# Squared-ReLU layer behind pooled attention and a soft mixture: joins spread over the steps, row additions moved to GpSimd, and another order of the first sixteen units

## The reference

```python
def _attn_ref(q, k, v):          # 8 batches, 8 heads, 576 tokens, head size 64
    k_p, v_p = ...               # keys and values averaged in groups of 8
    scores = scale * np.matmul(q, k_p.transpose(0, 1, 3, 2))
    ...
    return np.matmul(attn, v_p)

def _moe_ref(x, phi, w1, w2):    # soft mixture: x is (4608, 512), 32 slots in all
    logits = x @ phi
    ...
    return c @ slot_out          # c: (4608, 32), slot_out: (32, 512)

def _moe2_ref(x, w_in, w_out, s, b):   # w_in (512, 2048), w_out (2048, 512)
    h = x @ w_in
    r = np.maximum(h, 0.0)
    g = s * (r * r) + b
    return g @ w_out
```

## Time and profile before

| what | us |
|---|---|
| median of 3 runs | 681.96 (676.74 to 683.46) |
| profiled execution, its own time | 676.74 |
| its span | 674.9 |
| PE busy in the span | 637.7 (94%) |
| DVE, ACT, POOL busy | 480.2, 450.0, 126.1 |

### The profile page before, as it was taken

How to read it: one execution, slowest core, us unless ns; L and a number is a source line. 1 busy time by engine, 2 the same in 40 slices (tenths; PEclk the granted TensorE clock), 3 DMA queues, 4 the chain that set the end, 5 groups by cost and what they waited for, 6 DMA issues and landing times.

```text
span 674.9 us, 16536 instructions
## 1 busy us (share of the span) xinstructions
PE 637.7 (94%) x6466; PEld 550.2 (82%) x6466; DVE 480.2 (71%) x791; ACT 450.0 (67%) x753; POOL 126.1 (19%) x127
## 2 busy tenths in 40 slices
PE   7788999999998889989999999999999999999996
PEld 7566777776753247869999999999999999999996
DVE  5757575665344738875878777877787778777886
ACT  1576777776411279975777777777777777777771
POOL 3899786622110010002200000000000000000000
PEclk9799999999998999998999999999999999999999
DMA  9788969573589930000100000000000000000001
GB/s 336 229 265 295 362 211 404 164 306 128 190 311 432 424 140 1 1 0 16 64 18 32 18 18 29 22 24 16 31 16 31 16 31 16 31 16 31 17 33 48
DMA packets 25236, 80.49 MB, mean 119 GB/s; under 512 B 6496, under 2 KB 14688, under 8 KB 22368
## 3 DMA queue, kind: packets, MB, share of 16 engines
q1 hardware_dynamic: 25184, 79.76, 31.7%
HBM read 70.32 MB, written 9.44 MB: 118 GB/s over the span
## 4 chain that ended last, share of the span: by engine, by line
PE 40%; DVE 9%; issue 5%; ACT 3%; DVEq 0%; ACTq 0%
PE bank L1814 13%; PE bank L1816 12%; PE bank L1815 12%; DVE lo_sb L1303 3%; PE bank L1734 3%; ACT hi_sb L995 2%; DVE a_sb L1286 2%; DVE o_sb L1316 2%; DVE a_sb L1290 1%; PE bank L1776 1%; DVE a_sb L1292 0%; DVE o_sb L1355 0%; ACT r_sb L972 0%; ACT t_late L957 0%; DVE o_sb L1308 0%
## 5 line engine op out<-in xcount | busy, mean ns | idle before, releaser
L1303 DVE TENSOR_TENSOR lo_sb<-a_sb,hi_sb 128x896 fp32r<-128x896 f32 x128 | 140.2, 1096 | 66.2 <-ACT hi_sb L995 66.2
L995 ACT ACTIVATE hi_sb<-a_sb 128x896 fp32r<-128x896 f32 x128 | 121.9, 953 | 91.9 <-PE bank L1816 88.9
L1814 PE MATMUL bank<-w_hi,hi_sb 128*128 128x256 f32 x384 | 113.1, 294 | 7.0 <-DVE lo_sb L1303 6.9
L1815 PE MATMUL bank<-w_lo,hi_sb 128*128 128x256 f32 x384 | 108.8, 283 | 0.0
L1816 PE MATMUL bank<-w_hi,lo_sb 128*128 128x256 f32 x384 | 108.7, 283 | 0.0
L979 ACT ACTIVATE a_sb<-r_sb 128x512 f32<-128x512 f32 x144 | 91.1, 633 | 6.5
L972 ACT ACTIVATE r_sb<-bank 128x512 f32<-128x512 f32 x144 | 83.7, 581 | 2.9 <-PE bank L1734 2.9
L1814 PEld LDWEIGHTS bank<-w_hi,hi_sb 128*128 128x128 f32 x384 | 73.9, 192 | 11.7 <-DVE lo_sb L1303 10.9
L1815 PEld LDWEIGHTS bank<-w_lo,hi_sb 128*128 128x128 f32 x384 | 74.0, 193 | 0.0
L1816 PEld LDWEIGHTS bank<-w_hi,lo_sb 128*128 128x128 f32 x384 | 73.8, 192 | 0.0
L1816 PE MATMUL bank<-t_early,lo_sb 128*128 128x256 f32 x256 | 72.8, 284 | 0.0
(11 more groups left out here) (185 smaller groups left out, 1341.5 us busy)
## 6 DMA issues: line engine op xcount, KB each, us to landing
early_third<-in_moe_w_dram SPq DMA_DIRECT2D x6, 2048.0 KB, 13.8
kvbuf<-in_k_dram SPq DMA_DIRECT2D x12, 768.0 KB, 5.8
kvbuf<-in_v_dram SPq DMA_DIRECT2D x12, 768.0 KB, 6.7
out_dram<-o_sb SPq DMA_DIRECT2D x36, 256.0 KB, 2.3
qbuf<-in_q_dram SPq DMA_DIRECT2D x8, 1024.0 KB, 8.5
early<-in_moe_w_dram SPq DMA_DIRECT2D x4, 2048.0 KB, 12.2
late<-in_moe_w_dram SPq DMA_DIRECT2D x4, 2048.0 KB, 19.7
win_sb<-in_moe_w_in_dram SPq DMA_DIRECT2D x4, 1024.0 KB, 5.5
```

The costliest lines, as they stand in the source:

```text
L995: act.activation(hi_sb[:, n % 2, :], a_sb[:, n % ARING, P:2 * CH], ACT.Copy).then_inc(hi_ready, 1)
L1303: dve.tensor_tensor(lo_sb[:, n % 2, :], a_sb[:, n % ARING, P:2 * CH], hi_sb[:, n % 2, :].bitcast(F32), ALU.subtract).then_inc(lo_ready, 1)
L1814: pe.matmul(acc, hi, rhs_hi, start=opens, stop=False, skip_group_check=True)
L1815: pe.matmul(acc, hi, rhs_lo, start=False, stop=False, skip_group_check=True)
```

## The change

- **Joins and row additions.** The five joins of a half stand one behind each of steps 2 to 6 of the next half. The two additions of `row_b` leave DVE; POOL makes them, each when the join before it is done. In the last half DVE still makes the very last one.
- **Units.** In its round u ACT makes `relu` and `square` up to u + lead(u) before `high_easy(u)`, not behind it. PE issues h up to u + lead(u) + 2 behind unit u.
- **Combos.** POOL makes the first two sets, DVE the other six; the places of the sets' high and low parts move by a unit or two.
- **Row sum.** `sum_rows` goes from behind step 2 of half 0 to behind step 5, `scale_row` on ACT from step 4 to step 7, and what waits for the row on POOL with it.

```diff
-    POOL_COMBOS = 1
+    POOL_COMBOS = 2
...
             for m in range(MT):
-                sp.wait_ge(out_first, m + 1)
+                sp.wait_ge(out_ready, m + 1)
...
+            def add_row(m):
+                pool.tensor_tensor(o_sb[:, m, :], o_sb[:, m, :], row_b, ALU.add).then_inc(out_ready, 1)
+
+            def add_rows(c, odd, final):
+                pool.wait_ge(joined, c * JOINS + 3)
+                add_row(2 * odd)
+                if not final:
+                    pool.wait_ge(joined, c * JOINS + JOINS)
+                    add_row(2 * odd + 1)
...
-                pool.tensor_tensor(o_sb[:, m, :], o_sb[:, m, :], row_b, ALU.add).then_inc(out_first, 1)
+                add_row(m)
+            with pool.Fori(0, HALVES - 2, 2) as c:
+                add_rows(c, 0, False)
+                add_rows(c + 1, 1, False)
+            add_rows(HALVES - 2, 0, False)
+            add_rows(HALVES - 1, 1, True)
...
-                    if first and k == 4:
+                    if first and k == KP - 1:
                         scale_row()
...
-            high_at = {1: 0, 3: 1, 5: 2, 7: 3, 9: 4, 11: 5, 13: 6}
+            high_at = {1: 0, 2: 1, 4: 2, 6: 3, 8: 4, 11: 5, 14: 6}
             for u in range(F2C):
-                if u:
-                    high_easy(u)
                 while begun <= u + lead(u):
                     relu(begun, begun, bank[4 + begun % 2] if begun < F2C else bank[7], begun >= 2)
                     square(begun, begun, begun >= ARING)
                     begun += 1
+                if u:
+                    high_easy(u)
...
-                    if not first:
-                        for n in JOIN_AT[k]:
-                            join(c - 1, 1 - odd, n)
-                        if k in ADD_AT:
-                            add_row(c - 1, 1 - odd, ADD_AT.index(k))
+                    if not first and 2 <= k < 2 + JOINS:
+                        join(c - 1, 1 - odd, k - 2)
...
-            made_at = {1: 1, 3: 2, 5: 3, 7: 4, 9: 5, 11: 6, 13: 7}
-            low_at = {2: 0, 4: 1, 6: 2, 8: 3, 10: 4, 12: 5, 14: 6}
+            made_at = {2: 2, 4: 3, 6: 4, 8: 5, 10: 6, 13: 7}
+            low_at = {1: 0, 3: 1, 5: 2, 7: 3, 9: 4, 12: 5, 14: 6}
...
-            for n in range(3):
+            for n in range(JOINS):
                 join(HALVES - 1, 1, n)
-            join(HALVES - 1, 1, 3)
-            add_row(HALVES - 1, 1, 0)
-            join(HALVES - 1, 1, 4)
-            add_row(HALVES - 1, 1, 1)
+            dve.wait_ge(joined, HALVES * JOINS)
+            dve.tensor_tensor(o_sb[:, MT - 1, :], o_sb[:, MT - 1, :], row_b, ALU.add).then_inc(out_last, 1)
...
-                    while issued <= u + lead(u + 2) + 2:
+                    while issued <= u + lead(u) + 2:
                         hidden_at(issued)
                         issued += 1
...
-                    if first and k == 2:
+                    if first and k == 5:
                         sum_rows()
```

More of the change, by code:

```diff
@@ L356, in pooled_attention_soft_moe_squared_relu_kernel @@
         out_ready = sem("out_ready")
-        out_first = sem("out_first")
+        out_last = sem("out_last")
         o_dve = sem("o_dve")
@@ L734, in _ @@
                 for m in range(2):
-                    sp.wait_ge(out_ready, 2 * c + m + 1)
+                    if c == HALVES - 1 and m == 1:
+                        sp.wait_ge(out_last, 1)
+                    else:
+                        sp.wait_ge(out_ready, MT + 2 * c + m + 1)
                     sp.dma_start(tile_rows(MT + 2 * c + m), o_sb[:, 2 * (c % 2) + m, :]).then_inc(stored[2 * (c % 2) + m], 16)
@@ L1261, in combos @@
                 n = COMBOS * (k - POOL_COMBOS)
[L1262 to L1267, removed]
+                dve.wait_ge(t_hi_ready, k - 1)
+                dve.wait_ge(t_lo_ready, k - 1)
                 dve.tensor_tensor(t_raw_of(k, T1), raw_block(k, 0, 0), raw_block(k, 0, 1), ALU.subtract).then_inc(t_made, 1)
@@ L1345, in join @@
                 last.then_inc(joined, 1)
[L1347 to L1355, removed]
             def steps(c, odd, first, final):
```

## The result

The changed kernel takes 699.43 us (median of 4 runs, 696.41 to 702.8) where the kernel before took 679.93 us on the same chip (676.74 to 683.46): a ratio of 1.0287, with a 95% interval of 1.0211 to 1.0363. It is 19.5 us slower; the prediction said 20.9 us slower, 703 us.

What follows compares the result with a forecast made beforehand. PE, 94% busy, was taken as the bound, waiting only for DVE's low part; +6.3, +1.2, +11.5, -0.6 and +2.5 us on 676.74 gave 697.6 us, or 703 us against the median, range 690 to 712.

Steps and rivals of the forecast that it cites:

- Part 1: Joins and additions in the steady halves: PE waits for DVE, +0.42 us a half, +6.3 us over 15 halves.
- The first turn: Behind step 4, POOL's addition makes DVE stand 1.0 us after join 2; PE waits 0.7 us at step 5.
- the turn of 1.13 us: Alternative length of DVE's stand if POOL holds the port pair for its whole instruction; sum 2 us higher, not taken.
- The second turn: Behind step 6, POOL's addition stops DVE again; with join 3 delaying step 6's low part, 0.25 us are lost.
- Part 2: Four additions for the first tiles run into half 1: 2.4 us there, 1.15 us saved in half 0, net +1.2 us.
- Part 3: Units 6, 7, 9 and 10 stand in series because two order edits meet: 3.0 us each, +11.5 us.
- Part 5: PE's granted clock drops behind some of five new long waits: 1.5 drops taken, +2.5 us.
- Part 4: End of the kernel: POOL makes an addition that stood ahead of DVE's last one, -0.6 us.
- the signs named beforehand: Four 3 us unit waits, half 0 some 11 us later, token sums stretched 1 us, long half 1 wait, low clock.
- free turns: Rival: POOL's additions cost DVE nothing in the halves; about 686 us, chance 0.1.
- The threshold of 0.28 us: Behind an even step, a DVE stand below 0.28 us (0.95 - 0.67) would make POOL's addition cost PE nothing.
- the rival in which the clock falls with every long wait: PE's clock falls each time and POOL's additions stop DVE twice in full; 709 to 719 us, chance 0.17.

Runs made afterwards that it cites:

- spread_dve: The kernel before with joins one behind each of steps 2 to 6 and DVE's row additions behind steps 5 and 7; 669.18 us, ratio 0.9864.
- row_early: The changed kernel with the row sum as before: on PE behind step 2 of half 0, scaling on ACT in step 4; 699.62 us, ratio 1.0283.
- u_both: The changed kernel with both edits of the units' order undone, PE's issue of h and ACT's high part; 684.19 us, ratio 1.0081.
- u_pe: The changed kernel with only PE's issue of h as before; 688.16 us, ratio 1.0149.
- u_act: The changed kernel with only ACT's order in the units as before; 689.82 us, ratio 1.0168.
- tiny_adds: The changed kernel with POOL's additions in the halves cut to 8 of 512 columns, waits and counts kept; 686.43 us, ratio 1.012.
- early_set: spread_dve with ACT making the last set's high part at the end of unit round 15, ahead of step 0's high part; 664.82 us, ratio 0.979.
- pool_adds: The kernel before with the row additions on POOL and the joins where they were; 690.46 us, ratio 1.0178.
- pool_adds_odd: The kernel before with the row additions on POOL and all joins behind odd steps 1, 3 and 5; 670.14 us, ratio 0.9884.

## Why the prediction was right

The sign, the size and the places held: +20.9 us forecast, +19.5 us measured, and in the profiled executions +21.5 us. Term by term:

- **Part 1, the steady halves: right mechanism, too dear.** Forecast +0.42 us a half, measured +0.26 us (22.70 to 22.96), so some 3.9 us for 15 halves and not 6.3. The first turn measured 0.99 us (forecast 1.0; the turn of 1.13 us that the prediction weighs beside it doesn't show) and the wait at step 5 is 0.83 us on average (forecast 0.7). The second turn was forecast to cost 0.25 us through join 3; it cost nothing. In half 10 low part 5 ends at 545.75, PE starts at 545.80 and would begin step 7 two steps (5.52 us) later, at 551.32; low part 7 ends at 551.30. Join 3 did push low part 6, but the chain still arrived as PE did. And what the change removed was 0.62 us a half (22.70 - 22.09 of spread_dve), not 0.53.
- **Part 2, the four additions.** The wait before step 1 of half 1 is 2.71 us. The prediction had 2.4 us, from 3.3 us of turns; three turns of 1.0 us would give 3.0, and where its other 0.3 us comes from isn't said. The wait of 1.15 us in half 0 is gone, as forecast, and row_early against the changed kernel puts the net price of the late row sum at 1.3 us. From half 0 to half 2 the changed kernel takes 1.5 us more than the kernel before, with the first steady halves in it, where +1.2 us stood for the additions alone.
- **Part 3, the units.** Four waits of 3.02, 2.89, 3.02 and 2.80 us, 11.7 us in all; forecast 12.0, less 0.5 that they swallow. They are those of units 6, 7, 9 and 10. The other waits of the stretch come to 4.9 us in both kernels, so on balance nothing was swallowed. u_both, u_pe and u_act show that it takes both edits.
- **Part 5, the clock: too cheap.** Forecast 1.5 drops and 2.5 us; the clock fell behind all four waits between the units, and not behind the fifth long one, before step 1 of half 1. The first low part of half 0 comes 16.6 us later; 11.7 us of this are the waits, and PE began the stretch 0.95 us earlier, so the four drops cost the remaining 5.9 us, 1.5 us each. tiny_adds gives the same 1.5 us without a remainder; 1.7 us was reckoned. How many drops there are is partly chance: row_early, with the same four waits, has four, and tiny_adds has two.
- **Part 4, the end: right sign, half the size.** Forecast -0.6 us. In the three kernels whose additions stay on DVE (the kernel before, spread_dve, early_set) DVE ends 2.8 us behind PE's last matmul and the span 5.3 to 5.4 us behind it. In the nine with POOL's additions these are 2.3 us and 4.9 to 5.0 us. So some 0.3 us is gained; the longer wait in the last half takes it back.

Two errors of about 2.4 and 3.4 us, one in each direction, made the sum better than its terms: that much of the close result is luck. The mechanisms of parts 1 and 3 are shown by the experiments, and of the signs named beforehand the four waits, the stretched token sums, the long wait in half 1 and the low clock are all there; the first step of half 0 came 16.6 us later and not 11, for the clock. Of the rivals, free turns were refuted by tiny_adds and pool_adds. The threshold of 0.28 us, below which a turn would be free behind an even step, was not tested; pool_adds_odd shows another way to a free turn, placed where DVE waits anyway, with a period of 22.07 us. Of the rival in which the clock falls with every long wait, four of the five falls came, and the second meeting with the turn cost nothing.

## What to carry to other kernels

An engine with time to spare on average can still be the one that sets the pace: count what stands between the last thing that it can't start earlier and the next thing that is waited for, and put side work into the other gaps. Before moving work from VectorE to GpSimd, look in the trace for how long VectorE stands beside that very operation. When a table sets how far one engine runs ahead and another table which product the next engine wants first, compare the two index by index; one index is enough to put a pipeline in series.

## What the runs showed of the hardware that was not expected

- How long PE had waited doesn't tell whether its clock fell. In the twelve traces, from the first unit on, 40 waits of 2.36 us and more stand before a restart of PE, and the clock fell behind 24 of them. It fell behind ten of the twelve waits of 2.8 to 3.0 us between units (changed kernel and row_early four of four, tiny_adds two of four), behind three of the five of 2.7 us before step 1 of half 1, and behind eight of the eleven of 2.36 to 2.37 us before step 1 of half 0. Before unit 0 it fell behind two of six waits of 2.46 or 2.47 us and behind one of six of 3.11 to 3.58 us. Behind shorter waits, up to 1.92 us (u_act), it never fell.
- A join of 256 columns, which reads PSUM and one SBUF tile, ran 0.47 us beside a POOL addition (pool_adds_odd), as it does alone. The token sums and low parts, which read two SBUF tiles, stood: beside POOL's four additions in half 1 of the changed kernel a token sum of 0.68 us took 1.77 us and a low part of 1.09 us took 1.57 us.
- Executions of one kernel differ by more than several of the effects measured here: the kernel before took 674.43 to 687.52 us over all chips. The traces of the twelve kernels, whose first two layers are the same code, reach PE's first weight load for h between 242.19 and 247.82 us, with two to four stretches at the half clock ahead of it; whether that is the whole of the difference was not tested.
